# A doubled remainder ahead of the transposes, and a fifth matmul over 64 rows, in a windowed mix with an ELU MLP

## What is computed

```
B, S, D = 4, 4096, 192;  heads = 8;  K = 7;  d_ff = 2048
w = exp(weight_gen - max(weight_gen, -1))
w = w / (sum(w, -1) + 1e-9)                       # (B, S, 8, 7)
x_unf[b, s, k] = x_pad[b, s + k]                  # 6 rows of zeros ahead of each batch
x1 = einsum('bshk,bskhg->bshg', w, x_unf)         # (B*S, 192)
h = x1 @ w_in                                     # (16384, 2048)
g = where(h > 0, h, exp(min(h, 0)) - 1)
out = g @ w_out                                   # (16384, 192)
```

## Time and profile before

| | |
|---|---|
| device time, median of 3 runs | 1265.78 us (1263.91 to 1265.99) |
| span of the profiled execution | 1264.7 us |
| TensorE busy | 1207.9 us, 96% of the span, 6848 matmuls |
| weight loads busy | 1088.5 us, 86% |
| VectorE, ScalarE, GpSimd busy | 822.4 us (65%), 966.0 us (76%), 704.2 us (56%) |
| mean granted TensorE clock | 0.995 |

### The profile page before, as it was taken

How to read it: one execution, slowest core, us unless ns; L and a number is a source line. 1 busy time by engine, 2 the same in 40 slices (tenths; PEclk the granted TensorE clock), 3 DMA queues, 4 the chain that set the end, 5 groups by cost and what they waited for, 6 DMA issues and landing times.

```text
span 1264.7 us, 21620 instructions
## 1 busy us (share of the span) xinstructions
PE 1207.9 (96%) x6848; PEld 1088.5 (86%) x6848; DVE 822.4 (65%) x1453; ACT 966.0 (76%) x1897; POOL 704.2 (56%) x298
## 2 busy tenths in 40 slices
PE   2799999999999999999999999999999999999998
PEld 2699998989899898998989989898998989989998
DVE  7866666666566666666666566666666666666665
ACT  3588878778788787787778787787777877877886
POOL 8666654556645466554566545566454665545600
PEclk9899999999999999999999999999999999999999
DMA  7011011111011110011110011110111100110000
GB/s 223 32 48 49 14 36 47 47 48 47 1 47 47 48 47 31 18 47 48 47 48 20 28 47 47 48 47 1 47 47 48 47 21 27 47 48 13 13 14 13
DMA packets 17124, 52.13 MB, mean 41 GB/s; under 512 B 1944, under 2 KB 8212, under 8 KB 17040
## 3 DMA queue, kind: packets, MB, share of 16 engines
q1 hardware_dynamic: 17040, 51.36, 12.0%
HBM read 38.77 MB, written 12.58 MB: 41 GB/s over the span
## 4 chain that ended last, share of the span: by engine, by line
PE 88%; issue 5%; DVE 4%; ACT 3%; DMA 0%; SPq 0%; ACTq 0%; POOL 0%; DVEq 0%; POOLq 0%
PE slot L593 44%; PE acc L599 27%; PE acc L603 15%; ACT em L425 1%; DVE wout L503 1%; PE slot L581 1%; DVE g_lo L554 1%; ACT em L431 1%; DVE slot L548 1%; ACT g_hi L438 1%; PE slot L583 1%; DVE prod L471 0%; DVE prod L475 0%; DMA xwin<-in_x_dram 0%; SPq L242 0%
## 5 line engine op out<-in xcount | busy, mean ns | idle before, releaser
L548 DVE SCALAR_TENSOR_TENSOR slot<-em,slot 128x512 f32<-128x512 f32 x512 | 356.4, 696 | 419.2 <-ACT em L431 417.6
L599 PE MATMUL acc<-wout,g_hi 128*128 128x384 f32 x2048 | 469.7, 342 | 29.0 <-DVE g_lo L554 29.0
L425 ACT ACTIVATE em<-slot 128x512 f32<-128x512 f32 x512 | 305.4, 597 | 232.7 <-PE slot L593 183.8
L599 PEld LDWEIGHTS acc<-wout,g_hi 128*128 128x128 f32 x2048 | 369.2, 188 | 71.0 <-DVE g_lo L554 26.1
L554 DVE TENSOR_TENSOR g_lo<-slot,g_hi 128x512 fp32r<-128x512 f32 x511 | 350.1, 685 | 1.9
L431 ACT ACTIVATE em<-em 128x512 f32<-128x512 f32 x512 | 323.5, 632 | 16.3
L603 PE MATMUL acc<-wout,g_lo 128*128 128x192 f32 x2048 | 327.0, 266 | 0.9 <-DVE g_lo L554 0.9
L603 PEld LDWEIGHTS acc<-wout,g_lo 128*128 128x128 f32 x2048 | 312.0, 190 | 3.2 <-DVE g_lo L554 1.2
L331 POOL TENSOR_TENSOR prod<-xwin,probs 128x5376 f32<-128x5376 f32 (+1 forms) x32 | 308.1, 9628 | 8.1 <-POOL probs L317 6.5
L438 ACT ACTIVATE g_hi<-slot 128x512 fp32r<-128x512 f32 x511 | 298.1, 583 | 12.8 <-DVE slot L548 11.3
L593 PE MATMUL slot<-xt,win_hi 128*128 128x512 f32 x512 | 214.9, 420 | 2.7 <-DVE xt L516 2.7
(11 more groups left out here) (47 smaller groups left out, 585.1 us busy)
## 6 DMA issues: line engine op xcount, KB each, us to landing
xwin<-in_x_dram SPq DMA_DIRECT2D x30, 960.0 KB, 4.7
out_dram<-outs SPq DMA_DIRECT2D x32, 384.0 KB, 2.4
wg<-in_weight_gen_dram SPq DMA_DIRECT2D x32, 112.0 KB, 2.3
wout_raw<-in_moe_w_out_dram SPq DMA_DIRECT2D x4, 384.0 KB, 9.5
win_raw<-in_moe_w_in_dram SPq DMA_DIRECT2D x1, 768.0 KB, 6.5
win_rest_raw<-in_moe_w_in_dram SPq DMA_DIRECT2D x2, 384.0 KB, 8.6
xwin<-in_x_dram SPq DMA_DIRECT2D x1, 768.0 KB, 11.0
xwin<-in_x_dram SPq DMA_DIRECT2D x1, 384.0 KB, 3.7
```

What stands on the lines that cost most here:

```text
L425: nc.scalar.activation(em[:, i % 2, :], slot[s][:], ACT.Exp).then_inc(s_exp, 1)
L548: nc.vector.scalar_tensor_tensor(out=slot[s][:], in0=em[:, i % 2, :], scalar=0.0, in1=slot[s][:], op0=ALU.min, op1=ALU.max).then_inc(s_g, 1)
L599: pe.matmul(acc[j][:, 0:2 * d_model], g_hi[:, f % GBUFS, chunk(j)], wout[:, f, :], start=(f == 0), stop=False)
```

## The change

The 64 last mixed columns of a tile are written twice side by side into `mixed_rest`, so its transpose gives the same 64 rows in both halves of the partitions. There is one such transpose for each tile, not one for two tiles. One ScalarE instruction then copies the whole slot to `xt`, and one VectorE instruction makes all of `xt_lo`. The weights' remainder is one tile, `win_rest`, with the high part in partitions 0 to 63 and the low part in 64 to 127; the fourth matmul contracts it with the doubled high part of x over 128 rows, and the fifth contracts the high weights with the low part of x over partitions 0 to 63 alone.

```
-    XPARTS = 3
+    XPARTS = 1
...
-        win_rest_hi = sb("win_rest_hi", [P, d_ff], F32R)
-        win_rest_lo = sb("win_rest_lo", [P, d_ff], F32R)
+        win_rest = sb("win_rest", [P, d_ff], F32R)
...
-        mixed_rest = sb("mixed_rest", [P, 2, TILES, REST])
+        mixed_rest = sb("mixed_rest", [P, 2, TILES, 2, REST])
...
-        xt_lo = sb("xt_lo", [P, 2, N], F32R)
+        xt_lo = sb("xt_lo", [P, 2, 2, N], F32R)
...
+        def twice(t, tiles):
+
+            return t[:, :, P:].unsqueeze(2).broadcast_to([P, tiles, 2, REST])
...
                     cols = WIN_PARTS[1]
                     pool.wait_ge(s_whi, 3)
-                    nc.gpsimd.tensor_tensor(win_rest_lo[:, cols], win_rest_raw[:, cols],
-                                            win_rest_hi[:, cols].bitcast(F32), ALU.subtract).then_inc(s_plo, 1)
+                    pool.wait_ge(s_psoft, b.count(SOFTMAX, 1))
+                    nc.gpsimd.tensor_tensor(win_rest[REST:, cols], win_rest_raw[REST:, cols],
+                                            win_rest[REST:, cols].bitcast(F32), ALU.subtract).then_inc(s_plo, 1)
+                    pool.wait_ge(s_plo, 1)
...
-                nc.gpsimd.tensor_tensor(mixed_rest[:, q, first_tile:, :], one[:, :, P:], two[:, :, P:],
-                                        ALU.add).then_inc(s_add, 1)
+                nc.gpsimd.tensor_tensor(mixed_rest[:, q, first_tile:, :, :], twice(one, TILES - first_tile),
+                                        twice(two, TILES - first_tile), ALU.add).then_inc(s_add, 1)
...
-                nc.scalar.activation(xt[:, parity, 0, k * W:(k + 1) * W], slot[s][:, 0:W], ACT.Copy).then_inc(s_xhi, 1)
-                for t in range(PAIR):
-                    half_of = slice(t * REST, (t + 1) * REST)
-                    nc.scalar.activation(xt[half_of, parity, 1, k * W + t * P:k * W + (t + 1) * P],
-                                         slot[s][half_of, W:W + P], ACT.Copy).then_inc(s_xhi, 1)
+                nc.scalar.activation(xt[:, parity, :, k * W:(k + 1) * W],
+                                     slot[s][:].rearrange("p (a c) -> p a c", a=2), ACT.Copy).then_inc(s_xhi, 1)
...
-                nc.vector.tensor_tensor(xt_lo[:, parity, cols], slot[s][:, 0:W], xt[:, parity, 0, cols].bitcast(F32),
-                                        ALU.subtract).then_inc(s_xlo, 1)
-
-                for t in range(PAIR):
-                    half_of, other = (slice(a * REST, (a + 1) * REST) for a in (t, 1 - t))
-                    cols = slice(k * W + t * P, k * W + (t + 1) * P)
-                    nc.vector.tensor_tensor(xt[other, parity, 1, cols], slot[s][half_of, W:W + P],
-                                            xt[half_of, parity, 1, cols].bitcast(F32),
-                                            ALU.subtract).then_inc(s_xlo, 1)
+                nc.vector.tensor_tensor(xt_lo[:, parity, :, cols], slot[s][:].rearrange("p (a c) -> p a c", a=2),
+                                        xt[:, parity, :, cols].bitcast(F32), ALU.subtract).then_inc(s_xlo, 1)
...
-                rest = mixed_rest[:, parity, k * PAIR:(k + 1) * PAIR, :].rearrange("p t c -> p (t c)")
-                last = pe.transpose(slot[s][:, W:W + P], rest, ident[:])
+                for t in range(PAIR):
+                    rest = mixed_rest[:, parity, k * PAIR + t, :, :].rearrange("p a c -> p (a c)")
+                    last = pe.transpose(slot[s][:, W + t * P:W + (t + 1) * P], rest, ident[:])
                 last.then_inc(s_filled, 1)
...
-                        (win_hi[:, cols], xt_lo[:, parity, :]), (win_rest_hi[:, cols], xt[:, parity, 1, :]),
-                        (win_rest_lo[:, cols], xt[:, parity, 1, :]))):
+                        (win_hi[:, cols], xt_lo[:, parity, 0, :]), (win_rest[:, cols], xt[:, parity, 1, :]),
+                        (win_rest[0:REST, cols], xt_lo[0:REST, parity, 1, :]))):
                     last = pe.matmul(slot[s][:], w, v, start=(k == 0), stop=(k == 4))
```

More of the change, by code:

```diff
@@ L394, in _ @@
                 act.wait_ge(s_win[a], 48)
-                parts = ((win_hi, win_raw), (win_rest_hi, win_rest_raw))
+                parts = ((win_hi, win_raw), (win_rest, win_rest_raw))
                 for hi, raw in (parts if a == 0 else parts[::-1]):
@@ L486, in mix_vector @@
                 else:
-                    nc.vector.tensor_tensor(mixed_rest[:, q, 0:tiles, :], one_t[:, :, P:], two_t[:, :, P:],
+                    nc.vector.tensor_tensor(mixed_rest[:, q, 0:tiles, :, :], twice(one_t, tiles), twice(two_t, tiles),
                                             ALU.add).then_inc(s_vmix, 1)
@@ L494, in _ @@
             cols = WIN_PARTS[0]
[L495 to L498, removed]
+            dve.wait_ge(s_whi, 1)
+            nc.vector.tensor_tensor(win_lo[:, cols], win_raw[:, cols], win_hi[:, cols].bitcast(F32),
+                                    ALU.subtract).then_inc(s_wlo, 1)
+            dve.wait_ge(s_whi, 2)
+            nc.vector.tensor_tensor(win_rest[REST:, cols], win_rest_raw[REST:, cols],
+                                    win_rest[REST:, cols].bitcast(F32), ALU.subtract).then_inc(s_wlo, 1)
             def wout_rest(a):
```

## The result

The changed kernel takes 1443.72 us, the median of 4 runs (1441.74 to 1446.65), against 1265.85 us (4 runs, 1263.91 to 1265.99): a ratio of 1.1408, with a 95% interval of 1.1376 to 1.144. That is 178 us more. 1427 us had been forecast, with a range of 1270 to 1500.

A forecast was written before the change was run, and what follows sets the result against it. The prediction took TensorE to bound the kernel, busy 1207.9 of 1264.7 us. Its terms, 174 + 7 - 18 - 2 = +161 us, gave 1427 us, with a range of 1270 to 1500 us.

The forecast's parts named there:

- The mechanism: Fifth matmul of each first product: changing into its 64x128 tile and out again leaves weight loads uncovered, +174 us.
- c: Cost of the two changes of tile in each of 512 first products, estimated at 0.34 us.
- The discount for the way out: Leaving the fifth matmul's small tile: 0.15 us against 0.19 on entering, as the array holds only half the rows.
- the estimated 174: All changes of tile around the fifth matmul: 512 first products at 0.34 us, +174 us.
- The transposes: One more TensorE transpose in each of 64 x steps, 0.11 us each, +7.0 us on the chain.
- The terms put at nothing: X step: shorter ScalarE and VectorE work (21 and 20 us) and GpSimd's longer doubled add (18 us), all costed at nothing.
- What comes back at the turn: Loop's turn: ScalarE's gap stays, TensorE's longer lead shrinks 13 waits for `g_lo` by 1.36 us each, -18 us.
- The free change of tile: Rival at the fifth matmul: weight loads go ahead as before, only the transposes cost, 1273 us; chance 0.20.
- The rival for faster: Rival: free tiles, and the shorter x step on ScalarE and VectorE removes the turn's waits, down to 1252 us; chance 0.03.
- the start, put at -2: Start of the kernel: the first six or so first products run under VectorE's `wout` stall, -2 us.

The follow-up runs named there:

- Experiment 1: Changed kernel, but its fifth matmul contracts all 128 rows, so no change of tile is left: 1248.09 us, ratio 0.9868 to the kernel before.
- experiment 2: Kernel before, but its fifth matmul contracts only rows 0 to 63, nothing else of the change: 1444.38 us, ratio 1.1416.
- the hint: Kernel before, with a hint on every engine at the top of each loop pass that fetches the code behind the closing branch ahead: 1242.82 us, ratio 0.9813.
- experiments 11 and 12: Tiny ScalarE copies added: to Experiment 1's kernel, four per x step outside the loop and three inside, 1254.4 us; to the kernel before, twelve at the start, 1246.7 us.
- experiment 10: Experiment 1's kernel with three tiny ScalarE copies more in each x step inside the loop, none ahead of it: 1250.6 us.
- experiments 7 to 12: Tiny ScalarE copies added inside or outside the loop, to Experiment 1's kernel or, in the last, the kernel before: 1250.5, 1250.9, 1254.0, 1250.6, 1254.4, 1246.7 us.
- experiment 12: Kernel before, with twelve tiny ScalarE copies of a constant at the very start, nothing else: 1246.7 us, ratio 0.985.

## Why the prediction was right, and where it was wrong

**The mechanism held.** A change of tile keeps the next weights from being loaded ahead. From the fourth matmul's start to the fifth's load are 0.32 us (583.35 to 583.67), instead of 0.235 to the fifth matmul. Then the load itself stands open. I put that at 0.11 us, the step between the two small loads; the record of the fifth matmul, 0.50 us where its neighbours have 0.39 to 0.40, is longer by as much. 0.32 + 0.11 - 0.235 = 0.20 us for a change. The order alone of the same instructions moved the time by 205 us. The Trainium skill's TensorEngine Tiling (Array Packing), Key Properties, says that a change of the tiling mode drains TensorE, and that changing the tile within a mode doesn't; the runs agree with the first half, at 0.20 us each, as far as they reach: they show that the next load waits, and it begins at 583.67, 0.08 us before the record of the matmul ahead ends (583.35 + 0.40), an end that is modelled, so they can't show that nothing is left in the array by then. The second half was not tried (both small matmuls used the same tile).

**The size of c.** The working put 0.19 us on the way in and 0.15 on the way out, 0.34 together. Measured are 0.20 and 0.20, c = 0.40. The discount for the way out, that the array holds only half the rows then, was wrong: leaving the small tile costs as much as entering it. With 512 first products this is the 31 us between the estimated 174 and the measured 512 x 0.40 = 205 us. The estimate that the prediction made from the Trainium skill's TensorE: Matmul & The Clock Gate, with its drain of about 128 cycles on top of the open load, 164 us, was lower still.

**The transposes.** 0.11 us each, 7.0 us, were reckoned. Experiment 1 has x chunks of 2.74 us against 2.63 before, 0.11 more, as reckoned. In the changed kernel an x chunk stands 3.09 - 2.69 = 0.40 us over a plain one, against 0.33 before, only 0.07 more, 4 us in all: a change of tile ahead of transposes is a little cheaper (0.37 us for the first two instead of 0.22, so 0.15).

**The terms put at nothing.** ScalarE's copy of an x step took 0.59 us, VectorE's subtraction 0.68, and GpSimd's doubled add 1.29, all as reckoned, and none of the three engines is a part of the chunk's chain. Putting their own times at nothing was right; what the shorter instruction list of ScalarE did is another matter.

**What comes back at the turn.** This step failed, although the sum hides it. The working said that ScalarE's gap stays and that TensorE's longer lead covers 1.36 us of it at 13 turns, 18 us. In the changed kernel the gap isn't there at all. What the turns cost came back whole: 24.0 us, more than the 20.5 us in which the rows show TensorE waiting, since each restart costs some 0.3 us on top; and with them 1.6 us of the chunk at the lower clock. The lead would have covered most of it by itself, as experiment 2 shows, but the cause was ScalarE's shorter code, 12 instructions fewer ahead of the loop and 8 in it. The prediction read the gap as one "that no engine ends" and concluded that shorter work on ScalarE could not help; it never asked what fills such a gap. The row of the instruction queue was on the page, and four of its packets lie in the stretch around the turn, 568 to 576 us:

```profile
q14 instruction: 4, 0.03, 1.4%
```

**The rivals.** The free change of tile was given 1273 us. Experiment 1 is that case, and it took 1248: had tiles been free, the sign itself would have been wrong, by the step above. What fell of the rival itself is its premise: no load went ahead across a change of tile. The rival for faster had nearly the right price (20.5 us of waits against 7 of transposes: 1252 us where experiment 1 took 1248) and the wrong mechanism.

**The sum after the fact**, from the 43rd us of the spans on. Some 505 chunks grew by 0.395 us, 199.5; 62 x steps by 0.067, 4; the turns and the chunk at the lower clock gave back 25.6; the first three chunks behind VectorE's `wout` took 13.28 us instead of 8.64, 4.6 more; and the changed kernel was about one chunk further on by then (2.7): 199.5 + 4 - 25.6 + 4.6 - 2.7 = 180 us, which is the difference of the spans, 1444.7 - 1264.7. The forecast was +161, and that it came so near is in part luck, because its errors partly cancelled: the changes of tile came out 25.5 us above their term, the transposes 3 below, the turns and that chunk gave back 7.6 more, and the start, put at -2, came to 4.6 - 2.7 = +1.9. Of the 4.6, 1.2 are changes of tile, and the rest the clock:

```profile
43.00:55.00 12.00, 12.00 (x33) 8.43 (x32) 7.27 (x8) 4.93 (x9) 9.50 (x5) 0.51 0.08 33
```

The granted clock (third number from the end of this row of the changed kernel's windows) was 0.51, the lower of the two levels, 1.2 GHz, in this stretch right after the start's long waits; before it was 0.95 there. The two runs of the changed kernel with a mean clock of 1.0 took 1441.7 and 1442.0 us, those with 0.995 and 0.996 took 1446.7 and 1445.4. In the profiled execution the changes of tile in the rest of the kernel never lowered it.

## What to carry to other kernels

A matmul with fewer rows is not a cheaper one. Between matmuls of the full tile it costs 0.40 us more here than with the rows filled up, so fill the rows (with a term that does no harm, as in experiment 1) or put all small matmuls side by side, so that one pair of changes serves them all. When an engine stands in a gap that no other ends at a loop's branch, look at the instruction queue's packets before reckoning with the gap, and try the hint for the branch; any edit that shifts that engine's code can remove or bring back such a gap, and its 24 us can then be mistaken for the worth of the edit.

## What the runs showed of the hardware that was not expected

- ScalarE's fetch at the loop's turn follows the place of the code: 74 packets of 8 KB, or 9. The Trainium skill's Runtime: NRT & Kernel Launch, section on instruction fetch, says that code is held in two blocks of 256 instructions and that a taken branch to a block that isn't held forces a fetch. All rows of the table agree, if the borders lie at 193 to 196 and, 256 on, at 449 to 452: every loop that fetches touches three blocks, every other two. When I forecast experiments 11 and 12, I thought of blocks of 128; those fit as well, and no run tells the two apart.
- Why the gap was 3.90 us in the kernel before and 1.72 in experiment 10, with as many packets, was not settled.
- The mean plain chunk was 2.296 us before, 2.297 with the hint and 2.300 in experiment 1, but 2.307 in each of experiments 7 to 12, wherever ScalarE's loop starts (180, 192 or 204), and in 12 although its copies all run ahead of the loop. Over a kernel's plain chunks these 0.010 us are 4 to 5 us, about by how much experiment 12 stays behind the hint's 1242.8 (3.9 us). What only these six kernels have is one semaphore more and the small tile `spare`, declared ahead of `prod`, `mixed` and `xt`. Whether one of these makes the chunk longer was not tried.
- The four `wout` subtractions of VectorE at the start took 3.4 us in the mean after the change and 4.4 before, with the same work. Why was not tried.
